# Attention's output kept in SBUF past its loads, decay tables issued behind q and k, another order of seven products, and g_ln applied in the weight split

## The reference

```python
# 1. decayed linear attention, (B, H, S, D) = (4, 8, 768, 64)
for t in range(S):
    state = gamma[h] * state + outer(k[t], v[t])
    y[t] = (q[t] @ state) / sqrt(D)
x = y.transpose(0, 2, 1, 3).reshape(3072, 512)
# 2. first network, w_in 512x2048, w_out 2048x512
h = x @ w_in
x = where(h > 0, h, exp(min(h, 0)) - 1) @ w_out
# 3. second network, w_in 512x1024, w_out 1024x512
h = x @ w_in
solu = h * softmax(h)
out = (solu - mean(solu)) / sqrt(var(solu) + 1e-6) * g_ln @ w_out
```

## Time and profile before

| what | before |
|---|---|
| median of 3 runs | 867.68 us |
| the profiled execution | 866.43 us |
| its span | 864.6 us, mean granted clock 0.994 |
| PE / DVE / ACT / POOL busy | 839.2 / 575.7 / 417.4 / 406.1 us |
| bytes moved by DMA | 74.10 MB, mean 86 GB/s |

### The profile page before, as it was taken

One profiled execution on the slowest core, in us unless ns is written; L12 is line 12 of the kernel. 1 busy time (PEld: TensorE's weight loads), 2 busy tenths in 40 slices (PEclk: granted clock), 3 DMA queues, 4 the chain that ended last, 5 costly groups with the idle time before them and its releaser, 6 DMA issues.

```text
span 864.6 us, 12575 instructions
## 1 busy us (share of the span) xinstructions
PE 839.2 (97%) x4850; PEld 695.1 (80%) x4850; DVE 575.7 (67%) x842; ACT 417.4 (48%) x673; POOL 406.1 (47%) x450
## 2 busy tenths in 40 slices
PE   7988899999999999999999999979999999999998
PEld 5977688888888888888888888858878888888886
DVE  2587577776735465676455564896887777777773
ACT  3676565655435555544455554543333333333322
POOL 3668567575006666530267570695244444444200
PEclk9999999999999999999999999989999999999999
DMA  9999411013103011050201003502111111111001
GB/s 353 404 362 358 153 30 45 25 49 122 50 0 98 25 38 36 25 171 1 73 25 50 25 25 98 170 26 73 45 54 45 41 50 50 50 50 49 16 22 49
DMA packets 49643, 74.10 MB, mean 86 GB/s; under 512 B 3248, under 2 KB 23984, under 8 KB 49328
## 3 DMA queue, kind: packets, MB, share of 16 engines
q1 hardware_dynamic: 48864, 72.43, 24.8%
q10 hardware_dynamic: 720, 0.86, 0.3%
HBM read 56.50 MB, written 16.78 MB: 85 GB/s over the span
## 4 chain that ended last, share of the span: by engine, by line
PE 83%; DVE 8%; ACT 3%; DMA 3%; issue 2%; SPq 1%; POOL 0%; ACTq 0%; DVEq 0%
PE ps L674 9%; PE ps L678 9%; PE ps L675 9%; PE ps L627 8%; PE ps L629 8%; PE ps L628 8%; PE ps L775 5%; PE ps L777 5%; PE ps L776 5%; PE ps L686 4%; PE ps L688 4%; PE ps L687 4%; PE ps L761 2%; PE ps L604 2%; DMA v<-units_dram 2%; PE ps L579 2%
## 5 line engine op out<-in xcount | busy, mean ns | idle before, releaser
L486 POOL TENSOR_TENSOR u_lo<-u_raw,u_hi 128x256 fp32r<-128x256 f32 x168 | 147.9, 913 | 195.5 <-ACT u_hi L1103 195.5
L678 PE MATMUL ps<-g_lo,wd_hi 128*128 128x512 f32 x384 | 149.5, 389 | 2.0 <-DVE g_lo L887 2.0
L675 PE MATMUL ps<-g_hi,wd_lo 128*128 128x512 f32 x384 | 149.4, 389 | 0.0
L674 PE MATMUL ps<-g_hi,wd_hi 128*128 128x512 f32 x384 | 149.4, 389 | 0.0
L627 PE MATMUL ps<-x_hi,u_hi 128*128 128x512 f32 x336 | 131.4, 391 | 3.8 <-ACT p L1159 2.7
L628 PE MATMUL ps<-x_hi,u_lo 128*128 128x512 f32 x336 | 130.8, 389 | 0.0
L629 PE MATMUL ps<-x_lo,u_hi 128*128 128x512 f32 x336 | 130.7, 389 | 0.0
L481 POOL TENSOR_TENSOR u_raw<-u_raw 128x256 f32<-128x256 f32 x96 | 88.5, 922 | 14.3 <-DMA u_raw<-w_dram 8.1
L678 PEld LDWEIGHTS ps<-g_lo,wd_hi 128*128 128x128 f32 x384 | 72.1, 188 | 17.5 <-DVE g_lo L887 2.4
L675 PEld LDWEIGHTS ps<-g_hi,wd_lo 128*128 128x128 f32 x384 | 72.1, 188 | 15.0
L674 PEld LDWEIGHTS ps<-g_hi,wd_hi 128*128 128x128 f32 x384 | 72.1, 188 | 14.8
(11 more groups left out here) (87 smaller groups left out, 1522.7 us busy)
## 6 DMA issues: line engine op xcount, KB each, us to landing
u_raw<-w_dram SPq DMA_DIRECT2D x24, 512.0 KB, 3.7
k<-units_dram SPq DMA_DIRECT2D x12, 512.0 KB, 9.5
q<-units_dram SPq DMA_DIRECT2D x12, 512.0 KB, 8.2
v<-units_dram SPq DMA_DIRECT2D x12, 512.0 KB, 8.7
x_between<-x SPq DMA_DIRECT2D x24, 256.0 KB, 2.7
x_raw<-x_between SPq DMA_DIRECT2D x12, 512.0 KB, 3.6
out_dram<-y_sb SPq DMA_DIRECT2D x24, 256.0 KB, 2.0
kn<-units_dram SPq DMA_DIRECT2D x10, 512.0 KB, 9.1
```

What stands on the lines that cost most here:

```text
L486: nc.gpsimd.tensor_tensor(u_lo[n % 2][:, o, :], u_raw[n % 2][:, o, :], u_hi[n % 2][:, o, :].bitcast(f32), ALU.subtract).then_inc(ul_done, 1)
L674: nc.tensor.matmul(ps[:, bank + m, :], hi, g_hi[:, no % 3, :], start=(f == 0), stop=False)
L675: nc.tensor.matmul(ps[:, bank + m, :], lo, g_hi[:, no % 3, :], start=False, stop=False)
L678: last = nc.tensor.matmul(ps[:, bank + m, :], hi, g_lo[:, no % 3, :], start=False, stop=(f == NF1 - 1))
```

## The change

- `y_out_sb` has a buffer for each of the steps 4 to 11, over places that later hold g_hi, g_lo, raw wd 2 to 7 and wd_hi 2 to 5. SP stores them all after the last load of attention and after `load_u(1)`. Whatever is written there later waits for its stores: SP ahead of `load_wd(2)` for steps 7 to 9, ACT at `wd_split_hi(2)` for steps 10 and 11 and at the first `split_g_hi` for steps 4 to 6. ACT's wait for the last stores ahead of block 0 is gone. All wd from f = 2 on are loaded behind the stores.
- mask0 is issued by SP behind k and q of step 0, q_decay behind v of step 0; ACT issued both before. ACT starts with a copy of one column.
- The products of the first network run as 1-6-2-7-5-4-3; the operand lists follow. (Names M1 to M7 are places in the new order; P1 to P7 stay for the second network.)
- wd is split as 2i and 2i + 1 in unit i, from i = 1.
- The first half of x2 lies over slots 3 and 4 of `x_hi`; only `split_x_hi` of T4, the sixth, waits for its store. Sums stand at f = 3, 4, 5, 7, splits one f earlier for the first (hi at 5, lo at 6; the others as before).
- g_ln is applied in the split of w_out, in eight parts of 128x512: ACT copies with g_ln as scale, DVE subtracts with one `scalar_tensor_tensor`. `scale_w4` is gone. ACT does `split_x2_hi(1)` after f = 15. g_ln and the identity are loaded after block 0.

```diff
-        B11, B21, T3, B22, T1, T2, T4 = range(7)
+        B11, B21, T3, B22, T4, T1, T2 = range(7)
...
-              for h, at in enumerate((XH_AT, STASH_AT + 12 * K2))]
+              for h, at in enumerate((XH_AT + 6 * K2, STASH_AT + 12 * K2))]
...
+        y_at = [GH_AT, GH_AT + 4096, GH_AT + 8192, WLO_AT + 2 * K2, WLO_AT + 4 * K2, WLO_AT + 6 * K2,
+                WHI_AT + 2 * K2, WHI_AT + 4 * K2]
+        y_out_sb = {CB + s: place(f"y_att{s}", 1024, f32, at)[:, :].rearrange("p (n c) -> p n c", n=2)
+                    for s, at in enumerate(y_at)}
...
+        M1, M6, M2, M7, M5, M4, M3 = range(1, 8)
...
-        LEFT = [A11, S2, A12, S1, S3, A22, S4]
-        RIGHT = [B11, T2, B21, T1, T3, T4, B22]
+        LEFT = [A11, S2, A12, S3, S1, A22, S4]
+        RIGHT = [B11, T2, B21, T3, T1, T4, B22]
...
                 sp.dma_start(q_sb[slot], part(0)).then_inc(q_in[slot], 16)
+                if s == 0:
+                    sp.dma_start(mask0[:, :, :].rearrange("p h t -> p (h t)"),
+                                 tables[:, T_MASK0:T_MASK0 + H * C]).then_inc(mask0_in, 16)
                 sp.dma_start(v_sb[slot], part(3)).then_inc(v_in[slot], 16)
+                if s == 0:
+                    sp.dma_start(q_decay[:, :], tables[:, T_QDEC:T_QDEC + HH * C]).then_inc(q_decay_in, 16)
...
             for s in range(SLOTS, NS):
                 load_step(s)
-                if s - SLOTS >= CB:
-                    store_x(s - SLOTS)
             load_u(1)
-            for f in range(2, 8):
-                load_wd(f)
-            for s in range(NS - SLOTS, NS):
+            for s in range(CB, NS):
                 store_x(s)
-            sp.dma_start(gln_sb[:, :], g_ln).then_inc(gln_in, 16)
-            sp.dma_start(ident[:, :], tables[:, T_IDENT:T_IDENT + P]).then_inc(gln_in, 16)
-            sp.wait_ge(att_done, NS)
-            for f in range(8, NF1):
+            for s in range(CB + 3, CB + 6):
+                sp.wait_ge(x_stored[s], 32)
+            for f in range(2, NF1):
                 load_wd(f)
...
-                up(n, P2, X, A12, B21, False)
+                up(n, M2, X, A12, B21, False)
+                pe.wait_ge(h_summed, sums(n, U2))
+                up(n, M7, Y, S3, T3, False)
                 if i > 0:
                     pe.wait_ge(h_summed, sums(n - 1, H12))
-                up(n, P5, W, S1, T1, True)
-                pe.wait_ge(h_summed, sums(n, U2))
-                up(n, P7, Y, S3, T3, False)
+                up(n, M5, W, S1, T1, True)
                 between()
...
-            def w4_split_lo(k):
-                dve.wait_ge(w4_hi, k + 1)
-                part = slice(2 * k, 2 * k + 2)
-                nc.vector.tensor_tensor(wd_lo[:, part, :], wd_raw[:, part, :], wd_hi[:, part, :].bitcast(f32),
-                                        ALU.subtract).then_inc(w4_lo, 1)
+            def w4_split_lo(f):
+                dve.wait_ge(w4_hi, f + 1)
+                nc.vector.scalar_tensor_tensor(out=wd_lo[:, f, :], in0=wd_raw[:, f, :], scalar=gln_sb[:, f:f + 1],
+                                               in1=wd_hi[:, f, :].bitcast(f32), op0=ALU.mult, op1=ALU.subtract)\
+                    .then_inc(w4_lo, 1)
...
-                    if 4 <= f < 8:
-                        sum_x(blk + 1, f - 4)
-                    if 7 <= f < 14:
+                    if f in (3, 4, 5, 7):
+                        sum_x(blk + 1, (3, 4, 5, 7).index(f))
+                    if f == 6:
+                        split_x_lo(blk + 1, 0)
+                    if 8 <= f < 14:
                         split_x_lo(blk + 1, f - 7)
...
+                if no == 0:
+
+                    for s in range(CB, CB + 3):
+                        act.wait_ge(x_stored[s], 32)
...
-                if blk == 0 and i < NFP - 1:
-                    wd_split_hi(2 * i + 2)
+                if blk == 0 and i > 0:
+                    wd_split_hi(2 * i)
...
-            def w4_split_hi(k):
-                act.wait_ge(w4_scaled, k + 1)
-                part = slice(2 * k, 2 * k + 2)
-                nc.scalar.activation(wd_hi[:, part, :], wd_raw[:, part, :], ACT.Copy).then_inc(w4_hi, 1)
+            def w4_split_hi(f):
+                act.wait_ge(gln_in, 32)
+                act.wait_ge(w4_in[f // 2], 16)
+                nc.scalar.activation(wd_hi[:, f, :], wd_raw[:, f, :], ACT.Copy, scale=gln_sb[:, f:f + 1]).then_inc(w4_hi, 1)
...
                         if f == 8:
                             split_x2_hi(0)
-                        if f == 13:
-                            split_x2_hi(1)
                         if 11 <= f < 15:
-                            w4_split_hi(f - 11)
+                            w4_split_hi(2 * (f - 11))
+                            w4_split_hi(2 * (f - 11) + 1)
+            split_x2_hi(1)
             copy_p1(0)
```

## The result

The changed kernel took 854.27 us (median of 4 runs, 853.04 to 856.43), the kernel before 867.78 us beside it (866.13 to 868.86). The ratio is 0.985 (95% interval 0.982 to 0.988): 1.5% faster. The forecast was 855.2. The profiled execution took 853.04 us, its span is 851.2, against 866.43 and 864.6.

What follows compares the result with a forecast made beforehand. PE, busy 97% of the span, was taken as the bound, so only its stalls could be won: 3.2 + 2.7 + 6.6 = 12.5 us, from a median of 867.68 to 855.2 us, with 850.3 to 860.5 for 8 in 10.

Steps and rivals of the forecast that it cites:

- Attention: Attention steps 8 to 11: moving stores behind the last load removes three PE waits; -3.2 us, bounds 0 and -6.9.
- The opening edit: Attention steps 0 to 3: earlier table load, later mask0 and q_decay; lead lost at step 3's q; 0 us.
- The 0.5 us that I took off for VectorE's mask: Attention steps 8 to 11: VectorE's mask is late next, reducing the 3.66 us of waits by 0.5 us.
- Into block 0: From attention into block 0: 4.4 us lost before, mostly given back; -2.7 us, bounds -1 and -4.4.
- P4 doesn't wait (0.4 forecast): Start of block 0: VectorE has other work to do before U3, so P4 waits about 0.4 us.
- 1.3 + 0.4: Block 0: ScalarE's chain to the P1 copy ends 1.3 us after PE wants it; P4 waits 0.4 us.
- The turn: Turn into the second network: VectorE and POOL crowd relieved, clock stays at 2.4 GHz; -6.6 us, bounds -3 and -8.9.
- P2's wait: Turn, second network: PE stands 1.7 us at P2 for the copy of P1, behind x2_hi of unit 1.
- the chain on ACT: Turn: x2_hi of unit 1, after POOL's sums, stands ahead of the first P1 copy, which ends at 576.8.
- The other units: Other units, new product order: U2 ready after one product, 0.40 us spare; cost 0.
- What the prediction weighed beside it: Turn: VectorE's eight smaller subtractions may block POOL through shared SBUF ports, bringing unit 1's sums later than taken.
- The third rival: Turn wins only 3 us: x2_hi holds PE over 4 us and the clock falls; 858.8 us, chance 0.15.

Runs made afterwards that it cites:

- u0_behind_step4: Kernel after with the loads of u(0) and wd 0 and 1 behind step 4, its sums and split later; median 856.39 us.
- stores_in_loop: Changed kernel with the stores of steps 4 to 8 again among the loads; median 3.4 us up.
- order_15_74: Changed kernel with the products again in the order 1-6-2-5-7-4-3; median 0.8 us up, not told apart from the change's.
- u2_twice_old_order: Changed kernel with products in the old order 1-6-2-5-7-4-3 and VectorE making each U2 twice; 856.04 us.
- x2hi_1_at_13: Kernel after with ACT's split x2_hi(1) back at f = 13; 5.7 us more in the medians.
- tables_on_act: Changed kernel with mask0 and q_decay issued by ACT again ahead of everything; medians differ by 1.1 us, ranges overlap.
- x2_place_and_sums: Changed kernel with the place of x2's first half and the times of sums and splits as before; 3.3 us in the medians.
- p1_copy_and_exp_first: Kernel after with ACT's copy of P1 ahead of x2_hi(1) and its exponential of unit 0 ahead of x2_hi(2); median 854.47 us.
- g_ln_on_pool: Changed kernel with g_ln applied on POOL again (four scalings, plain copy and subtraction); price 6.2 us.
- u0_late_p1_exp: Kernel after with u(0), wd 0 and 1 loaded behind step 4 plus both ACT edits (P1 copy and exponential first); median not given.
- p1_copy_first: Changed kernel with ACT's copy of P1 ahead of x2_hi(1); lowest median, differing by 1.1 us with overlapping ranges.
- u2_twice_new_order: Changed kernel, new order, with VectorE making each U2 twice; 8.4 us more from first product to opening.

## Why the prediction was right

The span fell by 13.4 us where the working gave 12.5.

- **Attention, -3.2: -3.4.** First product at 82.16, forecast 82.4. The opening edit, 0, was right for its reason: the 0.9 us of lead at step 1 is gone at step 3, which waits for the bytes of its q (u0_behind_step4). Of the three waits that I laid to the stores, the two on `values` came back with them in stores_in_loop, 1.6 us in all; the one for q of step 11 didn't, so that part is read from the timelines alone. The 0.5 us that I took off for VectorE's mask is the 0.53 at 79.06.
- **Into block 0, -2.7: -3.0.** P4 doesn't wait (0.4 forecast) and P2 of unit 1 is 1.38 us later than 66 matmuls behind the first product, where 1.3 + 0.4 was forecast. Counted matmul by matmul from the first product, order_15_74, which has the old order and the rest of the change, is 2.28 us ahead of the kernel before behind the copy of P1 of unit 0, and 0.43 more at P2 of unit 1; the new order adds 0.27. That the 2.28 is ACT's wait for stores, now absent, and the 0.43 the two splits of wd that left unit 0, is read from the timelines; neither was undone alone.
- **The turn, -6.6: -7.2, and 0.2 given back at the end.** P2's wait is 1.80 us, forecast 1.7; the clock stayed at the 2.4 GHz level. That it stayed was partly luck: behind the same wait it fell in two of seven profiles, which cost 1.6 us (below). VectorE was ahead by more than I took: the last x_lo ends at 563.99, some 8 us earlier in the work than before, and it is 1.6 us clear of the opening. Behind that spare, the chain on ACT sets the end, as forecast. Three edits carry this term and none does it alone: undone one at a time they cost 6.2 (g_ln), 5.7 (x2_hi(1)) and 3.3 (place), 15 us for a term of 7, since each alone brings back one long wait, and with it the half clock.
- **The other units, 0.** True, with 0.40 us to spare; U2 0.6 us later would have cost 8.4 us of the gain.

What the prediction weighed beside it, VectorE and POOL in each other's way, can be read from the traces. This is VectorE and then POOL in the kernel before, at the four sums of unit 1:

```profile
569.84 2.38 DVE L887 TENSOR_TENSOR g_lo<-stash,g_hi 128x512 fp32r<-128x512 f32 x1
572.14 1.75 DVE L855 TENSOR_TENSOR x_lo<-x_raw,x_hi 128x1024 fp32r<-128x1024 f32 x1
573.81 1.75 DVE L929 TENSOR_TENSOR wd_lo<-wd_raw,wd_hi 128x1024 fp32r<-128x1024 f32 x1
575.48 1.21 DVE L887 TENSOR_TENSOR g_lo<-stash,g_hi 128x512 fp32r<-128x512 f32 x1
```

```profile
571.63 1.17 POOL L511 TENSOR_TENSOR x_raw<-x_raw 128x256 f32<-128x256 f32 x1
572.88 1.60 POOL L514 TENSOR_TENSOR x_raw<-x_raw 128x256 f32<-128x256 f32 x1
574.56 1.59 POOL L516 TENSOR_TENSOR x_raw<-x_raw 128x256 f32<-128x256 f32 x1
576.22 1.05 POOL L519 TENSOR_TENSOR x_raw<-x_raw 128x256 f32<-128x256 f32 x1
```

They end in turn, VectorE at 572.22, 573.89, 575.56 and 576.69, POOL at 572.80, 574.48, 576.15 and 577.27: each sum 0.6 us behind a VectorE instruction, each VectorE instruction 1.1 us (0.54 for 128x512) behind a sum. So a record holds the wait for the other engine's whole turn and then its own work. That is the rule of the Trainium skill (SBUF — State Buffer, Who interferes with whom): a VectorE instruction with two SBUF inputs contends with a GpSimd one that reads SBUF. The Trainium skill (SBUF — State Buffer, SBUF: two separate sides) says of this same pair that whichever starts first gets the shared ports for the whole instruction. The traces agree with both sentences. In them x_lo takes 1.21 us alone, 1.75 beside a POOL instruction of 128x256, and 2.91 beside a scaling, whose own turn is 1.75 us. U2, which has one operand in PSUM, takes its 0.69 us beside POOL too (307.24 in the kernel after). The third rival's eight chances did cost POOL time: two of the four sums of unit 1 came behind a new subtraction, with a turn of 0.55 us each. But in the kernel before each sum had come behind some VectorE instruction as well, the third behind an old subtraction with a turn of 1.08 us. So the sums took from 562.93 to 568.02, 5.1 us, where I had put 4.8 and the kernel before took 5.6.

## What to carry to other kernels

Where DMA is saturated, move stores that nobody waits for behind the last load, if there is room to hold their data; shifting loads among themselves mostly moved the wait here. Where two engines read SBUF side by side, look at the ends of their instructions: these show who waited for whom. Before an in-order queue is given an instruction that waits (x2_hi(1)), list what stands behind it and which engine wants that first. Measure the reserve of a tighter order by delaying its critical sum on purpose: 0.6 us cost 8.4 here, inside the 7 to 10 that the 0.40 us spare in the timeline had given.

## What the runs showed of the hardware

**PE stopped in the middle of a group without a wait.** `key_values` of step 10 is 32 matmuls, with all its semaphore waits ahead of the first. In eight of fourteen profiles PE stops for 0.15 to 1.80 us, always behind the sixth of them. Page part 3 counts packets of kind "instruction" on queue q8, and narrow windows give when one moved. First u2_twice_old_order, PE's timeline and then its DMA queues in 72.25 to 72.50 (packets, MB, share); then the same two views of the kernel after, the queues in 69.25 to 69.50:

```profile
72.54 0.45 PE L583 MATMUL ps<-v,kn 128*64 128x64 f32 x6
74.79 0.39 PE L583 MATMUL ps<-v,kn 128*64 128x64 f32 x6 [1.80 <-issue]
```

```profile
q8 instruction: 1, 0.02, 23.3%
```

```profile
72.62 1.15 PE L583 MATMUL ps<-v,kn 128*64 128x64 f32 x32
```

```profile
q8 instruction: 1, 0.02, 49.4%
```

Twelve profiles, in order of the packet:

```
packet at (within 0.25 us)   PE goes on at   stop     kernel
69.0 69.25 69.5 69.75        -               none     x2hi_1_at_13, after, tables_on_act, x2_place_and_sums
70.25                        72.97           0.15     p1_copy_and_exp_first
70.75                        73.18           0.16     g_ln_on_pool
71.0                         73.39           0.98     u0_behind_step4 (0.5 us earlier in its work)
71.25 71.25 71.25            73.65 to 73.87  0.7      u0_late_p1_exp, p1_copy_first, u2_twice_new_order
71.5                         73.88           0.98     order_15_74
72.25                        74.79           1.80     u2_twice_old_order
```

PE goes on 2.1 to 2.7 us behind the packet in all eight, and doesn't stop where it came early enough for that. In the kernel before and in stores_in_loop the packet moved at 70.50 and 72.00, and PE reached the group only at 74.03 and 75.19. I take it that PE's own code arrives late through DMA engines full of stores. No view names whose packet it is, but a count speaks for PE: from one packet of q8 to the next PE starts 255 matmuls and weight loads in the mean (four profiles, 38 spaces in each, means 254.5 to 255.7), whether the packets lie 6 us apart, as in attention, or 30, as in the first network; of VectorE's instructions it is 4 to 54. That the stores make it late wasn't tried apart. If so, keeping the stores together hands back 0 to 1.8 us from one execution to another; the first product lies anywhere from 81.8 to 84.2.

**A wait of 1.8 us sometimes halves the clock.** In the kernel after, u0_behind_step4, stores_in_loop and the two with U2 twice the clock stays at 1.00 behind a wait of 1.79 to 1.81 at P2; in tables_on_act and order_15_74 it falls to the 1.2 GHz level behind the same wait. PE and the windows in tables_on_act:

```profile
569.84 0.50 PE L672 MATMUL ps<-x_hi,u_hi 128*128 128x512 f32 x1 [1.79 <-ACT p L1191]
```

```profile
570.00:572.00 2.00, 2.00 (x6) 1.60 (x7) 1.79 (x3) 0.00 (x0) 2.00 (x3) 0.59 0.04 8
572.00:574.00 2.00, 2.00 (x6) 1.53 (x6) 0.00 (x0) 0.60 (x1) 2.00 (x4) 0.55 0.00 0
```

Opening to down is 8.88 to 8.92 us in the first group and 10.49 to 10.51 in the second: 1.6 us. Here at the turn it fell behind waits of 3.03, 3.81, 4.94 and 5.06 every time, behind 1.08 (three kernels) never. Elsewhere, too, the length of the wait alone doesn't decide: ahead of scores of step 3 PE stands 1.45 to 2.05 us in ten profiles, and the clock fell in one, stores_in_loop; and behind waits of 3.08 to 3.66 us in step 0 it stayed up in three (order_15_74, u0_behind_step4, u0_late_p1_exp). With the stop above, 1.6 + 1.8 us would be enough for the change's spread of 3.4; but one execution of each kernel was profiled, so that isn't shown. The kernels with the copy of P1 first spread over 1.2 to 1.9.
